# Attention output of batches 1 to 3 computed transposed: v and the state become the weights, the two heads take two column halves, and y is turned back one visit later

## The reference, cut to what matters

```python
for t in range(S):
    state = alpha[:, :, t, :, None] * state + np.einsum('bhd,bhe->bhde', k[:, :, t], v[:, :, t])
    y[:, :, t] = np.einsum('bhd,bhde->bhe', q[:, :, t], state)
```

## Time and profile before

| | us |
|---|---|
| median of 3 runs | 899.15 |
| lowest and highest run | 897.32, 919.35 |
| the profiled execution | 907.91 |
| its span, first to last instruction | 906.1 |
| TensorE busy in the span | 885.5 (98%) |
| VectorE, ScalarE, GpSimd busy | 451.3, 304.2, 200.0 |

### The profile page before, as it was taken

How to read it: one execution, slowest core, us unless ns; L and a number is a source line. 1 busy time by engine, 2 the same in 40 slices (tenths; PEclk the granted TensorE clock), 3 DMA queues, 4 the chain that set the end, 5 groups by cost and what they waited for, 6 DMA issues and landing times.

```text
span 906.1 us, 14525 instructions
## 1 busy us (share of the span) xinstructions
PE 885.5 (98%) x5372; PEld 853.6 (94%) x5372; DVE 451.3 (50%) x1077; ACT 304.2 (34%) x795; POOL 200.0 (22%) x330
## 2 busy tenths in 40 slices
PE   9998899999999999999999999999999999999998
PEld 6787899999999998998999999999999999999998
DVE  6658877657777568677452234222322242313121
ACT  2664555424544325554224242211221122112111
POOL 4626543103333023331003412000200020002000
PEclk9869999999999999999999999999999999999999
DMA  9924030040220040210045002000100010000000
GB/s 221 332 73 119 1 98 22 27 118 27 60 60 27 5 115 27 67 54 27 1 154 168 37 27 79 1 27 22 57 0 26 26 52 0 26 26 0 0 26 26
DMA packets 15001, 51.23 MB, mean 57 GB/s; under 512 B 1488, under 2 KB 6384, under 8 KB 13008
## 3 DMA queue, kind: packets, MB, share of 16 engines
q1 hardware_dynamic: 14368, 47.35, 17.4%
q0 software_dynamic: 576, 3.15, 0.9%
HBM read 41.07 MB, written 9.44 MB: 56 GB/s over the span
## 4 chain that ended last, share of the span: by engine, by line
PE 86%; DVE 7%; DMA 3%; issue 2%; ACT 1%; SPq 1%; DVEq 0%; POOL 0%; ACTq 0%
PE bank L1356 13%; PE bank L1358 13%; PE bank L1357 13%; PE pair L1356 12%; PE pair L1357 12%; PE pair L1358 12%; PE pair L1374 3%; DMA raw_a<-w_ch 3%; PE bank L1393 3%; PE bank L1402 2%; PE pair L1383 1%; PE bank L1398 1%; PE bank L1500 1%; PE bank L1363 1%; DVE stats L1135 1%
## 5 line engine op out<-in xcount | busy, mean ns | idle before, releaser
L1225 DVE SCALAR_TENSOR_TENSOR hl<-bank,hh 128x384 fp32r<-128x384 f32 x192 | 106.8, 556 | 330.3 <-ACT hh L787 330.3
L787 ACT ACTIVATE hh<-bank 128x384 fp32r<-128x384 f32 x192 | 94.3, 491 | 352.4 <-PE bank L1358 352.2
L1356 PE MATMUL bank<-nh,w1h 128*128 128x384 f32 x288 | 102.0, 354 | 0.5 <-DVE nl L1178 0.5
L1356 PE MATMUL pair<-w2h,hh 128*128 128x384 f32 x288 | 101.3, 352 | 0.0
L1356 PE MATMUL bank<-u2h,w3h 128*128 128x384 f32 x288 | 96.9, 336 | 0.9 <-DVE u2l L1312 0.9
L1356 PE MATMUL pair<-w4h,hh 128*128 128x384 f32 x288 | 97.2, 338 | 0.0
L1357 PE MATMUL pair<-w4l,hh 128*128 128x384 f32 x288 | 97.0, 337 | 0.0
L1357 PE MATMUL pair<-w2l,hh 128*128 128x384 f32 x288 | 96.9, 337 | 0.0
L1358 PE MATMUL pair<-w2h,hl 128*128 128x384 f32 x288 | 96.9, 336 | 0.0
L1358 PE MATMUL bank<-nh,w1l 128*128 128x384 f32 x288 | 96.8, 336 | 0.0
L1357 PE MATMUL bank<-nl,w1h 128*128 128x384 f32 x288 | 96.8, 336 | 0.0
(11 more groups left out here) (198 smaller groups left out, 1866.9 us busy)
## 6 DMA issues: line engine op xcount, KB each, us to landing
qkap<-qka SPq DMA_DIRECT2D x15, 1011.5 KB, 7.5
vt<-v SPq DMA_DIRECT2D x16, 288.0 KB, 8.1
raw_a<-w_ch SPq DMA_DIRECT2D x6, 768.0 KB, 7.2
mid<-u SPq DMA_DIRECT2D x8, 576.0 KB, 2.8
raw_b<-w_ch SPq DMA_DIRECT2D x6, 768.0 KB, 5.9
out<-u SPq DMA_DIRECT2D x8, 576.0 KB, 2.8
xr<-mid SPq DMA_DIRECT2D x7, 576.0 KB, 3.8
raw_t<-w_tok SPq DMA_DIRECT2D x2, 768.0 KB, 5.8
```

The costliest lines, as they stand in the source:

```text
L787: act.activation(hh[:, s % 4, :], bank[s % 2][:, 0:HALF], ACT.Relu).then_inc(s_hhi, 1)
L1225: dve.scalar_tensor_tensor(out=hl[:, s % 4, :], in0=bank[s % 2][:, 0:HALF], scalar=0.0, in1=hh[:, s % 4, :].bitcast(F32), op0=ALU.max, op1 ...
L1356: pe.matmul(out_ap, wh, rh, start=first, stop=False)
```

## The change

In batches 1 to 3, `attn_back` swaps the operands of each product, so that y comes out transposed, channels by tokens. v is now the weights and `at` streams, 128 columns per head; head 0's weights are 64 columns of v (its own 48 and 16 of head 1's) with output partitions 0 to 63, head 1's are 48 columns with output partitions 64 to 111. Where c is not 0, the state `dec` (now 128 columns wide, each head's block on the diagonal at rows and columns 0 and 64) is the weights and q streams, over all 112 output partitions. ScalarE copies the 112 x 128 result to a new tile `yt` (`attn_yt`). One visit later TensorE transposes `yt` back into columns 128 on of bank 7 (`attn_x`), ahead of that visit's own `attn_back`, and ScalarE copies from there into x, in pieces of 48 out of 64 columns. So each batch gets one more visit, 24, with nothing but the last transpose and copy; to make room, slot 20 leaves `PAUSES`, and visits 14 to 23 move one slot earlier. Batch 0 keeps its products (`first_back`) and its direct copy; it reads `dec` in its new layout.

```diff
-KV_AT, T_AT, Y_AT = 384, 256, 64
+KV_AT, T_AT, Y_AT, X_AT = 384, 256, 64, 128
-PAUSES = (0, 1, 9, 13, 20)
+PAUSES = (0, 1, 9, 13)
-VISIT = dict(zip([h for h in range(31) if h not in PAUSES], range(-2, STEPS)))
+VISIT = dict(zip([h for h in range(31) if h not in PAUSES], range(-2, STEPS + 1)))
...
-    dec = sb("dec", [P, 3, PW], o); o += 3 * PW * 4
+    dec = sb("dec", [P, 3, P], o); o += 3 * P * 4
+    yt = sb("yt", [P, P], o); o += P * 4
...
     def visited(a, k):
-        return a * (STEPS + 2) + k + 3
+        return a * (STEPS + 3) - (1 if a else 0) + k + 3
-    def y_of(a, k):
-        first = 0 if a else Y_AT
-        return visit_bank(a, k)[:, first:first + PW]
+    def x_of(a, k):
+        if a == 0:
+            return visit_bank(a, k)[:, Y_AT:Y_AT + PW].rearrange("p (h n) -> p h n", h=2)
+        return visit_bank(a, k)[:, X_AT:X_AT + P].rearrange("p (h n) -> p h n", h=2)[:, :, 0:D]
...
 # ScalarE
             def attn_x(a, k):
                 if k == 0 and a:
                     act.wait_ge(s_ua, a * UA)
+                act.wait_ge(s_vis, visited(a, k + 1 if a else k))
+                act.activation(x[:, k % NC, (k // NC) * PW:(k // NC + 1) * PW].rearrange("p (h n) -> p h n", h=2),
+                               x_of(a, k), ACT.Copy).then_inc(s_x, 1)
+            def attn_yt(a, k):
                 act.wait_ge(s_vis, visited(a, k))
-                act.activation(x[:, k % NC, (k // NC) * PW:(k // NC + 1) * PW], y_of(a, k), ACT.Copy).then_inc(s_x, 1)
+                act.activation(yt[0:PR, :], visit_bank(a, k)[0:PR, 0:P], ACT.Copy).then_inc(s_yt, 1)
...
                 attn_krt(a, k + 2)
-                if k >= 0:
-                    attn_x(a, k)
+                if a and 0 <= k < STEPS:
+                    attn_yt(a, k)
+                if k >= (1 if a else 0):
+                    attn_x(a, k - 1 if a else k)
                 decay(a, k + 2)
...
 # TensorE
             def attn_back(a, k):
                 c, vb = k % NC, vt[unit_buffer(a, k // NC)]
-                y = y_of(a, k)
                 pe.wait_ge(s_at, a * STEPS + k + 1)
                 for h in range(2):
-                    if a:
-                        mm = pe.matmul(y[:, h * D:(h + 1) * D], at[:, k % 2, h, :], vb[:, c, h * D:(h + 1) * D],
-                                       start=h == 0, stop=c == 0 and h == 1)
...
+                    rows = slice(64 * h, 64 + D * h)
+                    values = vb[:, c, D * h:D * h + rows.stop - rows.start]
+                    mm = pe.matmul(visit_bank(a, k)[rows, 0:P], values, at[:, k % 2, h, :], start=True, stop=c == 0)
                 if c:
                     for h in range(2):
                         pe.wait_ge(s_dec[h], a * STATES + state_index(k - 1) + 1)
-                    mm = pe.matmul(y, q_of(a, k), dec[0:PR, k % 3, :], start=False, stop=True)
+                    mm = pe.matmul(visit_bank(a, k)[0:PR, 0:P], dec[0:PR, k % 3, 0:PR], q_of(a, k), start=False, stop=True)
                 return mm
+            def attn_x(a, k):
+                pe.wait_ge(s_yt, (a - 1) * STEPS + k + 1)
+                return pe.transpose(visit_bank(a, k)[:, X_AT:X_AT + PR], yt[0:PR, :], ident[0:PR, 0:PR])
...
-                if was >= 0:
-                    pe.wait_ge(s_x, a * STEPS + was + 1)
+                if was >= (1 if a else 0):
+                    pe.wait_ge(s_x, a * STEPS + was + (0 if a else 1))
...
-                if k >= 0:
-                    mm = attn_back(a, k)
+                if a and k >= 1:
+                    mm = attn_x(a, k - 1)
+                if 0 <= k < STEPS:
+                    mm = attn_back(a, k) if a else first_back(k)
```

More of the change, by code:

```diff
@@ L225, in program @@
               "at_ready", "state_ready", "visit_done", "x_ready"])
+    s_yt = sem("y_copied")
     s_dec = [sem(f"state_decayed{h}") for h in range(2)]
@@ L681, in decay @@
                     r = head_rows(1)
-                    act.activation(dec[r, k % 3, D:PW], st[r, (k - 1) % 3, D:PW], ACT.Copy, scale=chunk_decay(k, r)
+                    act.activation(dec[r, k % 3, r], st[r, (k - 1) % 3, D:PW], ACT.Copy, scale=chunk_decay(k, r)
                                    ).then_inc(s_dec[1], 1)
@@ L1384, in attn_kv, with first_back @@
                                  stop=True)
+            def first_back(k):
+                c, vb = k % NC, vt[k // NC]
+                pe.wait_ge(s_at, k + 1)
+                for h in range(2):
+                    first = Y_AT * (1 - h)
+                    both = visit_bank(0, k)[:, first:first + 2 * ASIDE].rearrange("p (g n) -> p g n", g=2)[:, :, 0:D]
+                    mm = pe.matmul(both, at[:, k % 2, h, :], vb[:, c, :], start=h == 0, stop=c == 0 and h == 1)
+                if c:
+                    for h in range(2):
+                        pe.wait_ge(s_dec[h], state_index(k - 1) + 1)
+                    states = dec[0:PR, k % 3, :].rearrange("p (h n) -> p h n", h=2)[:, :, 0:D]
+                    mm = pe.matmul(x_of(0, k), q_of(0, k), states, start=False, stop=True)
+                return mm
             def attn_back(a, k):
                 c, vb = k % NC, vt[unit_buffer(a, k // NC)]
-                y = y_of(a, k)
                 pe.wait_ge(s_at, a * STEPS + k + 1)
                 for h in range(2):
-                    if a:
-                        mm = pe.matmul(y[:, h * D:(h + 1) * D], at[:, k % 2, h, :], vb[:, c, h * D:(h + 1) * D],
-                                       start=h == 0, stop=c == 0 and h == 1)
[L1395 to L1398, removed]
+                    rows = slice(64 * h, 64 + D * h)
+                    values = vb[:, c, D * h:D * h + rows.stop - rows.start]
+                    mm = pe.matmul(visit_bank(a, k)[rows, 0:P], values, at[:, k % 2, h, :], start=True, stop=c == 0)
                 if c:
```

## The result

| | us |
|---|---|
| first comparison: before, median of 4 | 898.39 (897.32 to 919.35) |
| after, median of 4 | 928.38 (923.72 to 931.65), ratio 1.0298 [1.0229, 1.0367] |
| the profiled execution after, its span | 931.65, 929.8 |
| repeat on another occasion: before, median of 18 | 899.85 (897.68 to 921.07) |
| after, median of 6 | 915.26 (913.22 to 923.61), ratio 1.0175 [1.0109, 1.0240] |

In both comparisons after is slower, but by 30 us and by 15. Sorted by the granted clock of the run there is one answer: at 1.00 before takes 897.4 to 899.0 and after, in the one run at 1.00, 913.2: **some 15 us**. All four runs of the first comparison had 0.974 to 0.983, so that a part of each ran at the lower clock; in the profiled one it lies in batch 0.

A forecast was written before the change was run, and what follows sets the result against it. TensorE, busy 98%, was taken to bound batches 1 to 3. Visits add 17.4 us, 2 us are absorbed, the other parts cost zero: net +15 on a median of 899.15 gives 914 us, range 890 to 929.

The forecast's parts named there:

- Streaming columns, halves with gaps, side by side: TensorE, v product of a visit: heads run together, array empties before and after, 0.58 us; 914 us had chance 0.58.
- one after another: v product of a visit: gaps, and the second head's passes follow the first's, 0.21 us more; 930 us, chance 0.19.
- both rivals without gaps: v product of a visit, loads hidden: heads together 890 us, chance 0.13; heads in turn 905 us, chance 0.10.
- Visits without a state: The 12 visits with c = 0 in batches 1 to 3: each +0.30 us on TensorE.
- What is absorbed: TensorE's waits in the first visits of each batch take up 2 us of the added time.
- Sum of the visits: TensorE, batches 1 to 3: 60 visits at +0.23 and 12 at +0.30, in all +17.4 us.
- Slots: Slots 20 to 30, visits moved one earlier: TensorE's work the same, VectorE's norm split at most 1.7 us, taken as zero.
- ScalarE: The added copies into `yt` make ScalarE 19 us busier, but cost zero, with 1.5 us to spare before TensorE's transpose.
- Batch 0: Batch 0 keeps its products and reads `dec` in pieces of 48 out of 64: no cost.
- Block 3 unchanged: Work after the batches: the second MLP was to stay unchanged, with nothing added.
- The likeliest outcome, within 2%: Whole kernel: time between 881 and 917 us, chance 0.66.
- the 0.32 that I had left for slower: Whole kernel: slower by more than two per cent, chance 0.32.

The follow-up runs named there:

- shifted by 512 bytes: The kernel before with 512 bytes left free behind the state tile, no instruction changed: 900.25 us, ratio 0.9997.
- whole-width experiment: The changed kernel with batch 0's old state tile and copy, v's products over all 112 output partitions, heads mixed: 915.59 us, ratio 1.0139.
- the shifted kernel: The kernel before with 384 bytes left free behind the state tile and 512 behind the small tiles, no instruction changed: 904.77 us, ratio 1.0030.
- The filled kernel before: The kernel before with one unused filler product in all 24 visits of batch 0 instead of the first five: 901.65 us, ratio 1.0007.
- the late splits: ScalarE's weight splits and GpSimd's low parts moved to later visits of batch 0: kernel before 903.28 us (0.9989), changed kernel 917.37 us (1.0150).

## Why the prediction was right, step by step

The median on record, 928.38, lies 14 us above the 914 that was forecast and inside the range of 890 to 929 by 0.6 us, through the clock in batch 0, which the prediction doesn't speak of: that is luck. What its sum is worth shows at the full clock. Measured between two profiles at a clock of 1.00 throughout, after (repeat) and before (shifted by 512 bytes, with the times of before): spans 911.4 and 896.1, **+15.3**. By stretches:

| stretch | before | after | more | forecast |
|---|---|---|---|---|
| to batch 0's flips | 49.79 | 50.06 | 0.3 | 0 |
| batch 1 (flips to flips) | 109.42 | 113.38 | 4.0 | 5 |
| batch 2 | 125.83 | 129.71 | 3.9 | 5 |
| batch 3 | 126.09 | 130.09 | 4.0 | 5 |
| to block 3's first product | 119.97 | 120.58 | 0.6 | 0 |
| block 3 | 364.97 | 367.59 | 2.6 | 0 |

- *Streaming columns, halves with gaps, side by side*: right. From the trace of after, gap 0.09, the passes with their first load and the gap behind them 0.36, the state's load that nothing covers 0.10: 0.55 us (forecast 0.58). The state product takes 0.31 - 0.10 = 0.21 as forecast, the transpose 0.08 to 0.10 (0.11). Together +0.19 where +0.23 was forecast. The rival *one after another* (930) falls by the starts 6 ns apart; both rivals without gaps fall by the whole-width experiment. That the first median came near 930 is no support for the first of them: the time lies in batch 0, not in the visits.
- *Visits without a state*: over-sized, 0.30 forecast and 0.18 measured. Behind them the turn of the keys follows the halves, and the next product starts 0.08 behind the turn (0.05 before): the uncovered load that I had added whole is 0.03 there.
- *What is absorbed*: 7.4 - 5.6 = 1.8 us, forecast 2.
- *Sum of the visits*: 60 x 0.19 + 12 x 0.18 = 13.6, less 1.8, plus 1.2 for the wait at the flips, less some 0.6 that the new addresses give back (an estimate, 0.2 a batch, from batches 2 and 3 of the shifted kernel): 12.4. Measured 11.8.
- *Slots*: cost zero held around slot 20. But I wrote that the sums and folds behind the last copy of x start no earlier against TensorE. They start later: slot 30 has one transpose instead of a visit, so its MLP products begin 0.03 us behind that (309.51 to 309.54) and not 0.59 behind the start of the visit (293.04 to 293.63), VectorE isn't ready any sooner (its split `hl`, its sums of x and the flips follow each other behind the last `mlp_in` product as before), and TensorE waits 0.3 to 0.6 us at the flips for the first of these sums, which ends at 311.54 where the flips start at 311.64.
- *ScalarE*: cost zero held; no wait of TensorE for `yt` is in the rows. ScalarE is busy 13 us more and not 19, since the copies of a visit start 0.16 apart and overlap in the record.
- *Batch 0*: 0.3 us at full clock. In the first comparison the clock cost another 15 us (928.38 against 913.2; in the profiled run batch 0's flips start 19 us later than in the repeat); before has such drops too, 34 times in 86.
- *Block 3 unchanged*: the step that failed, a cost put at nothing. Its instructions are, their operands' addresses aren't: 2.6 us, and 0.6 ahead of it.

So +15 came out right with two errors that cancel, which is luck: the batches were costed 3 us too dear, and 3.2 us of addresses were not foreseen. The mechanism inside the visits, halves with gaps and side by side, is what the trace shows. The likeliest outcome, within 2%, is what the runs at full clock show (1.7%); the repeat's interval reaches past 2%, and the first comparison lies wholly above it, in the 0.32 that I had left for slower.

The Trainium skill has the recipe of two column tiles in "TensorEngine Tiling (Array Packing)", section Performance Considerations; its section Overview (Theoretical Speedup) gives up to twice the speed for a dimension of at most 64. The trace shows the doubling in the streaming, 0.21 us (0.36 less the load of 0.05 and the gap of 0.09 to 0.10) instead of 0.43, and shows it spent on gaps and uncovered loads.

What stays open: why four runs of four lost the clock in the first comparison and two of six in the repeat (six of ten, against 34 of 86 before, can be chance, but nothing excludes a part of the edit in batch 0); what in the addresses slows the products; and what more than a wait it takes for the clock to fall. A wait alone is not enough: the filled kernel before waited 1.3 us once, on GpSimd, and kept 1.00, and the profiles without fillers that kept 1.00 have waits of 2.1 to 2.5 us near 96 us. No version beat the kernel before.

## What to carry to other kernels

Don't split the array for one short f32 product between whole-width ones: here the two gaps and the uncovered load cost more than running side by side gives (0.10 us a visit). Whether a longer run of split products pays was not tried. Before blaming an edit for a large change in time, sort the runs by granted clock and compare stretch by stretch at the same clock. And when a tile grows, what lies behind it moves: leave the same bytes free in the old kernel once, and see what the place alone costs.

## What was not expected of the hardware

- The place of the operands changes TensorE's pace slightly: in block 3 the products with the last MLP's weights (w3, w4) start 174 to 177 ns apart in the kernel shifted by 384 bytes and 173 to 174 in the kernel before, by medians; block 3 takes 2.6 us of 365 more.
- In the six profiles with a long drop of the granted clock to 0.50 (24 to 48 us), TensorE's longest wait between 12 and 40 us was 0.9 to 2.0 us, and the drop began between 0.1 us ahead of its end and 1.9 us behind it. In the three profiles without fillers that kept 1.00 the longest wait there was 0.4 us. With the late splits it was 0.4 to 0.6; there a wait of 2.0 us ends between 48 and 50 us, with a short drop (3 to 7 us) that begins between 1.1 us ahead of its end and 2.0 us behind it.
- A VectorE instruction on 112 x 4 elements took 1.88 us instead of 0.17 while a GpSimd product of 1.81 us ran, and ended with it (47.30 and 47.27 us).
- Two column groups of f32 products, two passes each, run side by side (starts 146.821 and 146.827, 146.974 and 146.981 us), which no row of before showed.
